# A fused attention and two-mixer kernel: the weight product on other steps with a buffer of its own, four weight pieces before the first step, VectorE's mixer work on other steps

## What is computed

```
attention: 8 heads of width 64
  scores = q k^T / 8, causal; bias = min(cum_k - cum_q, 0), cum = cumsum(max(s, 0))
  x = softmax(scores + bias) v                       -> 576 x 512 per batch
first mixer:
  gate = sigmoid(5-tap causal convolution of x over tokens)
  x = (gate * (x w_val)) w_out
second mixer:
  h = relu(x w_in); u, v = halves of h
  v_n = (v - mean v) / sqrt(var v + 1e-6)            (over the 512 features)
  out = (u * (w_spatial v_n + b_spatial)) w_out2
```

## Time and profile before

| what | value |
|---|---|
| median of the three runs | 577.82 us |
| the profiled execution | 578.55 us |
| its span, first to last instruction | 576.7 us |
| outside the span | 1.85 us |
| mean granted TensorE clock | 0.967 |
| ScalarE / VectorE / GpSimd busy | 57% / 63% / 44% of the span |
| first score matmul starts | 11.31 us |
| head 10 starts (step 50) | 155.9 us |
| the last batch is alone on the core from about | 505 us |

### The profile page before, as it was taken

The page is one execution under the profiler, slowest core; times in us unless marked ns, Lnnn a source line. Parts: engine busy times, 40 slices in busy tenths (PEclk is TensorE's granted clock), DMA queues, the critical chain, the costliest instruction groups (busy, mean ns, idle before and its releaser), DMA issues.

```text
span 576.7 us, 10409 instructions
## 1 busy us (share of the span) xinstructions
PE 519.3 (90%) x3472; PEld 453.6 (79%) x3472; DVE 365.4 (63%) x726; ACT 329.7 (57%) x844; POOL 254.8 (44%) x247
## 2 busy tenths in 40 slices
PE   1378887876999899999999999999998999999998
PEld 1256665654897699998986899988876999997997
DVE  5355766887767756676767666759576656565240
ACT  2466765675566565576665655666665645633322
POOL 2444643435457654633656635334666444003000
PEclk9998889975899999999999999999999999999999
DMA  5765454332333333344333222343333320200002
GB/s 138 215 185 142 136 135 107 83 97 70 85 84 83 84 84 78 77 114 115 96 86 84 73 72 57 93 136 95 84 91 76 84 63 13 73 20 2 1 2 82
DMA packets 46887, 50.34 MB, mean 87 GB/s; under 512 B 24881, under 2 KB 29137, under 8 KB 46834
## 3 DMA queue, kind: packets, MB, share of 16 engines
q1 hardware_dynamic: 46834, 49.68, 32.7%
HBM read 25.83 MB, written 4.95 MB: 53 GB/s over the span
## 4 chain that ended last, share of the span: by engine, by line
PE 44%; DVE 4%; ACT 2%; issue 1%; POOL 1%; DMA 0%; ACTq 0%; SPq 0%; POOLq 0%
PE mix L1039 23%; PE attn_o L1007 5%; PE attn_o L1039 4%; PE score L1039 4%; PE turned L998 3%; PE score L977 2%; PE score L978 1%; DVE u_t L895 1%; DVE neg_max L849 1%; DVE u_t L933 1%; PE score L979 1%; DVE pt_lo L867 1%; PE score L986 1%; PE score L987 1%; DVE stats L925 1%
## 5 line engine op out<-in xcount | busy, mean ns | idle before, releaser
L721 ACT ACTIVATE prob<-score,neg_max 128x128 f32<-128x128 f32 (+4 forms) x159 | 90.3, 568 | 108.7 <-DVE neg_max L849 108.2
L867 DVE TENSOR_TENSOR pt_lo<-turned,pt_hi 128x128 fp32r<-128x128 f32 (+4 forms) x160 | 77.5, 489 | 67.2 <-ACT pt_hi L730 66.5
L849 DVE TENSOR_REDUCE neg_max<-score 128x1 f32<-128x128 f32 (+4 forms) x159 | 85.1, 535 | 38.1 <-PE score L979 32.1
L730 ACT ACTIVATE pt_hi<-turned 128x128 fp32r<-128x128 f32 (+4 forms) x160 | 66.6, 435 | 42.2 <-PE turned L998 40.7
L634 POOL TENSOR_TENSOR q<-raw,raw_hi 64x576 fp32r<-64x576 f32 x32 | 46.0, 1438 | 86.3 <-issue 69.4
L977 PE MATMUL score<-k,q 68*128 68x256 f32 (+2 forms) x128 | 54.3, 424 | 29.3 <-ACT prob L721 14.4
L998 PE MATMUL turned<-ident,prob 128*128 128x128 f32 (+1 forms) x480 | 73.6, 276 | 7.1 <-DVE pt_lo L867 7.1
L1007 PE MATMUL attn_o<-pt_hi,v_hl 128*128 128x256 f32 (+2 forms) x224 | 66.7, 314 | 6.2 <-DVE pt_lo L867 6.2
L998 PEld LDWEIGHTS turned<-ident,prob 128*128 128x128 f32 (+1 forms) x480 | 50.0, 150 | 15.7 <-issue 14.5
L406 POOL TENSOR_TENSOR act_b<-u_t,act_b 128x288 fp32r<-128x288 f32 x48 | 41.1, 860 | 42.7 <-ACT act_b L795 42.1
L1039 PE MATMUL mix<-ws_hl,act_a 128*128 128x288 f32 (+1 forms) x405 | 59.2, 298 | 0.0
(11 more groups left out here) (150 smaller groups left out, 1039.0 us busy)
## 6 DMA issues: line engine op xcount, KB each, us to landing
q<-raw_hi SPq DMA_DIRECT2D x64, 144.0 KB
k<-raw_hi SPq DMA_DIRECT2D x64, 144.0 KB
raw<-in_q SPq DMA_DIRECT2D x32, 144.0 KB, 2.7
raw<-in_k SPq DMA_DIRECT2D x32, 144.0 KB, 2.8
r_bc<-r_dram SPq DMA_DIRECT2D x32, 144.0 KB, 2.9
out<-work SPq DMA_DIRECT2D x32, 144.0 KB, 1.8
v_raw<-in_v SPq DMA_DIRECT2D x32, 128.0 KB, 2.2
u_t<-in_moe_w_in SPq DMA_DIRECT2D x7, 256.0 KB, 3.5
```

The costliest lines, as they stand in the source:

```text
L721: act.activation(prob_view(i), score_view(g, i), ACT.Exp, bias=neg_max[p][0:rows[i], i:i + 1], accum_out=row_sum[p][0:rows[i], i:i + 1]).t ...
L730: act.activation(pt_view(pt_hi, i), turned_view((g + i) % 2, i), ACT.Copy).then_inc(pt_hi_done, 1)
L849: dve.tensor_reduce(neg_max[g % 2][0:rows[i], i:i + 1], score_view(g, i), AX_X, ALU.max, negate=True).then_inc(max_done, 1)
L867: dve.tensor_tensor(pt_view(pt_lo, i), turned_view((g + i) % 2, i), pt_view(pt_hi, i).bitcast(F32), ALU.subtract).then_inc(pt_lo_done, 1)
```

## The change

1. **Weight product.** w_out now goes into `ws_hl`, the buffer of w_spatial, and `act_a` is free for x_hi, whose wait for the product is gone. The 32 parts stand on a list of steps, 6, 7, 9, 11, and then every step from 12 to 47 but i = 0 and step 17.
2. **Weights.** w_spatial's five pieces go behind the product, with w_out2's four, to steps 48 to 56 (low parts one step later), in four staging tiles used in turn. The first four pieces are loaded right behind the load of head 0 (`first_weights`), and split before step 0; `more_weights` now loads seven pieces instead of four. The bias row is rounded at step 7 instead of 3.
3. **scale_q** of a head moves one step later, from i = 4 to i = 0 of the next head.
4. **Mixer tables.** Taps, tanh, x_hi, statistics, normalisation and splits of v have other steps, and the eviction of v moves from the lead to the tail of its step.

```diff
@@ -44,17 +44,16 @@
     def put(at, step, *unit):
         at.setdefault(length + step, []).append(unit)
 
-    for n, step in enumerate((-14, -12, -11, -9, -7, -7, -6, -4, -3, -2, -1, -1, 1, 2, 3) if first else
-                             (-22, -21, -19, -17, -16, -12, -11, -9, -7, -6, -2, -1, 1, 2, 3)):
-        put(tail, step, "tap", n // TAPS, n % TAPS)
-    for t, step in enumerate((7, 7, 8, 9, 9)):
-        put(tail, step, "tap", 3, t)
-    for c, step in enumerate((-4, -1, 4, 10)):
-        put(lead, step + 1, "tanh", c)
-    for c, step in enumerate((0, 2, 4, 6)):
+    for c, step in enumerate((1, 3, 4, 6)):
         put(lead, step, "x_hi", c)
         put(tail, step, "x_lo", c)
-
+    for n, step in enumerate((-17, -16, -16, -14, -12, -11, -11, -9, -7, -6, -2, -2, -1, 1, 3) if first else
+                             (-22, -21, -21, -17, -16, -12, -11, -11, -9, -7, -2, -2, -1, 1, 3)):
+        put(tail, step, "tap", n // TAPS, n % TAPS)
+    for t, step in enumerate((7, 8, 8, 9, 9)):
+        put(tail, step, "tap", 3, t)
+    for c, step in enumerate((-5, -4, 5, 10)):
+        put(lead, step, "tanh", c)
     step = 8
     for side in range(2):
         for m in range(4):
@@ -65,10 +64,10 @@
     for j in range(5):
         put(lead, step, "mm", ("v", j, 0), 0)
         put(lead, step + 1, "mm", ("v", j, 0), 1)
-        put(lead, step + 1, "evict", ("v", j, 0))
-        put(tail, (17, 19, 21, 23, 26)[j], "stats", j)
-        put(tail, (19, 21, 23, 24, 28)[j], "norm", j)
-        put(tail, (20, 22, 24, 26, 29)[j], "split", ("v", j, 0))
+        put(tail, step + 1, "evict", ("v", j, 0))
+        put(tail, (18, 21, 22, 24, 26)[j], "stats", j)
+        put(tail, (21, 23, 24, 26, 28)[j], "norm", j)
+        put(tail, (23, 24, 25, 28, 29)[j], "split", ("v", j, 0))
         step += 2
     for n, u_step in enumerate((0, 0, 1, 2, 3, 4, 5, 5)):
         side, m = divmod(n, 4)
@@ -303,25 +302,26 @@
                 PIECES.append((view[:, k, :], P, length, to, k * length))
 
         for kk in range(NC):
-            PIECES.append((wo_view[:, kk, :], P, C, act_a, kk * C))
+            PIECES.append((wo_view[:, kk, :], P, C, ws_hl, kk * C))
             PIECES.append((wi_view[:, kk, C:2 * C], P, C, act_b, kk * C))
         cut_by(wi_view[:, :, 0:C], NC, C, w2_hl)
         WV_PIECE = len(PIECES)
         cut_by(wv_view, NC, C, wv_hl)
+        LATE_PIECE = len(PIECES)
         cut_by(w_spatial[0:FULL * P, :].rearrange("(k p) t -> p k t", p=P), FULL, S, ws_hl)
         PIECES.append((w_spatial[FULL * P:S, :], LAST, S, ws_hl, FULL * S))
-        W2_PIECE = len(PIECES)
         cut_by(w2_view, NC, C, w2_hl)
         NCOMB = 2 * NC
         STAGES = SLOTS + 2
         FIRST_LOADS = 4
         WEIGHTS_FROM = 2
-        COMB_FROM = 8
-        W2_FROM = COMB_FROM + NC * NCOMB
+        COMB_STEPS = [6, 7, 9, 11] + [n for n in range(12, H * NT + 8) if n % NT != 0 and n != 17]
+        assert len(COMB_STEPS) == NC * NCOMB
+        LATE_FROM = H * NT + 8
 
         def staged(n):
             _, r, length, _, _ = PIECES[n]
-            tile = n % STAGES if n < W2_PIECE else (SLOTS, SLOTS + 1, SLOTS - 1, SLOTS - 2)[n - W2_PIECE]
+            tile = n % STAGES if n < LATE_PIECE else (SLOTS, SLOTS + 1, SLOTS - 1, SLOTS - 2)[(n - LATE_PIECE) % 4]
             return u_t[0:r, tile, 0:length] if tile < SLOTS else work[tile - SLOTS][0:r, 0:length]
 
         block = ctx.enter_context(nc.Block())
@@ -422,16 +422,16 @@
                         call(unit[0], b, b == B - 1, *unit[1:])
 
             def weights(step):
-                for n in range(len(PIECES)):
-                    at = WEIGHTS_FROM + n if n < W2_PIECE else W2_FROM + n - W2_PIECE
+                for n in range(FIRST_LOADS, len(PIECES)):
+                    at = WEIGHTS_FROM + n if n < LATE_PIECE else LATE_FROM + n - LATE_PIECE
                     if step == at:
                         call("weights_hi", n)
                     if step == at + 1:
                         call("weights_lo", n)
 
             def comb(step):
-                n, kk = divmod(step - COMB_FROM, NC)
-                if 0 <= n < NCOMB:
+                if step in COMB_STEPS:
+                    n, kk = divmod(COMB_STEPS.index(step), NC)
                     call("comb_mm", n, kk)
                     if kk == NC - 1:
                         call("comb_evict", n)
@@ -464,15 +464,13 @@
                     call("invert_sums", g - 1)
                 if i == 0 and 0 <= g - 2 < NH:
                     call("combine", g - 2)
-                if step == 0:
-                    call("scale_q", 1)
+                if i == 0 and g + 1 < NH:
+                    call("scale_q", g + 1)
                 if i == (0 if g == 0 else 1) and g + 1 < NH:
                     call("split_qk", g + 1)
                     call("place_qk", g + 1)
                 if step == 0:
                     call("more_weights")
-                if i == 4 and g + 2 < NH:
-                    call("scale_q", g + 2)
                 if i == 2 and g + 2 < NH:
                     call("load_qk", g + 2)
                 if i == 3 and 0 <= g - 1 < NH:
@@ -486,6 +484,7 @@
 
             call("setup")
             call("load_qk", 0)
+            call("first_weights")
             call("cumulate")
             call("scale_q", 0)
             call("keep_cumulated")
@@ -494,13 +493,16 @@
             call("load_qk", 1)
             call("later_setup")
             call("load_v", 0)
+            for n in range(FIRST_LOADS):
+                call("weights_hi", n)
+                call("weights_lo", n)
             for step in range((B - 1) * H * NT + H * NT + length):
                 mixer(0, step)
                 comb(step)
                 attention(step)
                 early(step + 1)
                 weights(step)
-                if step == 3:
+                if step == 7:
                     call("bias_rows")
                 mixer(1, step)
 
@@ -520,19 +522,19 @@
                     sp.wait_ge(cum_split, n + 1)
                     sp.dma_start(cum_dram[:, n, :], words(t[1][0:NH, :])).then_inc(stored, 16)
 
-            def later_setup():
+            def first_weights():
                 for n in range(FIRST_LOADS):
                     load_weights(n)
 
             def more_weights():
-                for n in range(FIRST_LOADS, STAGES):
+                for n in range(FIRST_LOADS, FIRST_LOADS - 1 + STAGES):
                     load_weights(n)
                 sp.dma_start(r_bc[0:1, :], b_spatial.rearrange("(a t) -> a t", a=1)).then_inc(b_loaded, 16)
 
             def load_weights(n):
                 view, r, length, _, _ = PIECES[n]
-                if n >= W2_PIECE:
-                    wait_pieces(sp, W2_PIECE)
+                if n >= LATE_PIECE:
+                    wait_pieces(sp, max(LATE_PIECE, n - 3))
                 elif n >= STAGES:
                     wait_pieces(sp, n - STAGES + 1)
                 sp.dma_start(staged(n), view).then_inc(w_loaded[n % STAGES], 16)
@@ -546,11 +548,13 @@
 
             def weights_lo(n):
 
-                if 0 < n <= W2_PIECE - STAGES:
+                if FIRST_LOADS <= n <= LATE_PIECE - STAGES:
                     load_weights(n - 1 + STAGES)
-                if n == W2_PIECE - 1:
-                    for late in range(W2_PIECE, len(PIECES)):
+                if n == LATE_PIECE - 1:
+                    for late in range(LATE_PIECE, LATE_PIECE + 4):
                         load_weights(late)
+                if LATE_PIECE <= n < len(PIECES) - 4:
+                    load_weights(n + 4)
 
             def load_qk(g):
                 wait(sp, lo_made, 2 * g)
...
@@ -691,7 +695,7 @@
                 act.wait_ge(w_loaded[n % STAGES], 16 * (n // STAGES + 1))
                 if n == WV_PIECE:
                     act.wait_ge(b_placed, 32)
-                if n == W2_PIECE:
+                if n == LATE_PIECE:
                     act.wait_ge(comb_done, NCOMB)
                 act.activation(to[0:r, 0, at:at + length], staged(n), ACT.Copy).then_inc(w_hi_done, 1)
 
@@ -742,8 +746,6 @@
 
             def x_hi(b, alone, n):
                 act.wait_ge(x_done, NC * b + n + 1)
-                if b == 0 and n == 0:
-                    act.wait_ge(comb_done, NCOMB)
                 if b > 0:
                     act.wait_ge(unit_done, NU * (b - 1) + LAST_SPATIAL + 1)
                 act.activation(chan(act_a, 0, n), x_t[:, n, PAD:PAD + S], ACT.Copy).then_inc(x_hi_done, 1)
@@ -885,7 +887,7 @@
                     dve.wait_ge(x_done, NC * b + n + 1)
                     dve.wait_ge(const_loaded, 16)
 
-                    wait_pieces(dve, W2_PIECE if b == 0 else len(PIECES))
+                    wait_pieces(dve, LATE_PIECE if b == 0 else len(PIECES))
                     if NC * b + n >= SLOTS:
                         before, m = divmod(NC * b + n - SLOTS, NC)
                         dve.wait_ge(lo_done, NS * before + SPLIT[("spatial", m, 1)] + 1)
@@ -954,7 +956,7 @@
```

(6 more changed lines are left out.)

4 lines of the change are left out of this document (2 added, 2 removed).

## The result

The changed kernel takes 578.88 us (median of 20 runs, 576.69 to 581.61), the kernel before, on the same chips, 575.98 (20 runs, 574.70 to 580.02). The ratio of after to before is 1.0041, interval [1.0023, 1.0059]. The forecast was 566.0 with 557 to 575: the time lies outside it. By the bound of 1% the change makes no difference; inside that bound it is slower rather than faster. The same file run again later in the study gave 1.0020 [0.9996, 1.0043].

A forecast was written before the change was run, and what follows sets the result against it. TensorE was taken as the bound from head 12 on, and the ring of scores to transposes in the first 156 us. Terms -1.5, -4.0, -5.7, +1.2 and -2.5 sum to -12.5: 578.55 to 566.0 us, range 557 to 575.

The forecast's parts named there:

- The batches from head 12 on: Three batches: TensorE's waits at the v units shrink, a new one comes; net -0.8 us each, -2.5 in all.
- The new wait on the eviction of v tile 4: Step 66 of each batch: second u product waits 1.3 us for ScalarE's eviction behind the attention, scores queued behind it.
- Heads 2 to 7: Weight pieces, waits of q's scaling and some product parts leave these heads: -4.0 us (0 to -8).
- The rival of a falling clock: Heads 4 to 7: thinned product lets TensorE's clock fall, +18 us in place of -4.0, total 588.0; chance 0.07.
- Heads 8 and 9: Both at head 5's 12.4 us plus two val products, 28.2 in place of 33.9: -5.7 us (-2 to -9).
- "more than that" rival: Clock stays at its upper level, heads 2 to 9 all run like head 5: -15.6 us there, total 560.1; chance 0.20.
- The late pieces: Heads 9 to 11: nine pieces in steps 48 to 57 make TensorE wait now and then, +1.2 us (0 to 5.5).
- the late pieces hold VectorE: Heads 9 to 11: POOL's five pieces each hold VectorE, +5.5 us in place of +1.2, total 570.3; chance 0.15.
- the ring: Loop of scores, row maximum, exponential and transposes, said to set the pace in the first 156 us.
- The start: Heads 0 and 1: bias row's wait goes, head 2's load becomes late; row maximum near 27, -1.5 us (-4 to +1).
- The sum: Whole kernel: -1.5 - 4.0 - 5.7 + 1.2 - 2.5 = -12.5 us, from 578.55 to 566.0.
- The signs: Right: head 8 under 14 us, 9 under 15.5, 12 starting near 173. Wrong: head 10 over 16.5, a batch over 122.

The follow-up runs named there:

- e6: The changed kernel with the eviction of v back in the lead of its step: 573.50 us, 0.9955 of the kernel before.
- e9: The changed kernel with three of the seven pieces and the bias row loaded at step 3, behind head 2's q and k: 577.79 us, 1.0011.
- e1: The changed kernel with the product's parts of steps 6, 7, 9 and 11 moved to steps 15, 17, 20 and 25: 573.33 us, 0.9939.
- e2: The changed kernel with seven of nine late pieces rounded and split over 16 columns only, so its result is not right: 572.59 us, 0.9929.
- e5: The changed kernel with the product at steps 8 to 39 and the late pieces at 40 to 48: 572.15 us, 0.9934.
- e7: The kernel before with tables, scale_q and start changed, but product and w_spatial's pieces where they were: 577.48 us, 1.0022.
- e12: The kernel before with the new mixer tables alone, but v evicted in the lead as before: 575.27 us, 0.9963.
- e4: The kernel before with only the scaling of q moved one step later: 579.47 us, 1.0049.
- e3: The kernel before with the new mixer tables alone, eviction of v in the tail: 584.43 us, 1.0134.
- e13: The kernel before with the new mixer tables and the scaling of q at i = 0, nothing else: 577.42 us, 1.0010.
- e8: The kernel before with only the four early pieces, seven loads at step 0 and the bias row at step 7: 578.74 us, 1.0043.
- e10: The changed kernel with product at steps 10 to 41, late pieces at 42 to 50, v evicted in the lead, q and k loaded ahead of three pieces: 566.93 us, 0.9819.

## Why the forecast was wrong

The total was forecast at -12.5 us; the medians say +2.9, the ratio +2.4 (+1.3 to +3.4). Point by point, in the forecast's own parts:

**The batches from head 12 on: right in kind.** The new wait on the eviction of v tile 4 was named and sized at 1.3 us; the first reads 1.68, the others 1.2. The net of -0.8 a batch reads -0.8 in the second and -1.1 in the third. My own terms (-1.0, half of -1.9, +1.3) give -0.65, so the close agreement is partly luck. The first came out at +1.6 against a forecast of -0.8: it starts with a stretch at the lower clock from 182 to 186 us, as the second profile of the same file, e6 and e9 do. In e1, e2, e5 and e7 the stretch of lower clock is missing, and the group takes 120.7 or 120.8. The wait of 2.2 us on an exponential ahead of it is no explanation, since e1 has it too (2.25). What sets it off I can't say from these runs. What I had not seen is how much better the same tables do without the late eviction (e6, -1.5 a batch; e12, -9.2 in all).

**Heads 2 to 7: right, and undersized.** Forecast -4.0, measured -7.6 and -6.1. The move of scale_q alone gives -3.7 there (e4), but beside the new tables it gives next to nothing (83.4 in e3, 83.2 in e13); most of the gain comes with the move of the product and the pieces (82.6 in e7, 76.7 in after). In the working, half of what stands between head 3 and head 5 is 1.6 and not 1.3; with 0.9 for head 4 the term stays where it was. The rival of a falling clock is out: heads 4 to 7 read 1.00.

**Heads 8 and 9: the step that failed most.** The forecast said "I take both at head 5's 12.4", -5.7 us. They took 34.0 (33.9 before), at 0.75 of the granted clock. The clock stayed down from 118 to 121, 128 to 138 and 141 to 145 us. Running both heads at head 5's length and running them at full clock were told as one term, as if the extra product parts would bring the clock with them; in head 8 TensorE was busy for 12.2 of 15.4 us and still read 0.75. Nor did I name what came ahead of the val products: at 137.71 ScalarE's x_hi waited 2.58 us for GpSimd's x_t, which I had listed only against the "more than that" rival. Identical code in these heads gave 34.0 and 32.9 us, and nearly identical code 31.7, 30.5, 30.3 and 33.2 (e1, e2, e6, e9). The windows of heads 8 and 9 of after and of e6:

```profile
116.80:150.80 34.00, 29.18 (x149) 24.02 (x149) 24.52 (x43) 19.44 (x48) 13.93 (x9) 0.75 0.29 75
```

```profile
119.80:150.10 30.30, 25.31 (x148) 20.47 (x149) 23.11 (x43) 19.35 (x48) 13.96 (x9) 0.89 0.33 85
```

TensorE is not busy for 4.8 us in the one and 5.0 in the other, and for 5.0 to 5.2 in the four others. What differs is the granted clock: 0.75 goes with 34.0 us, 0.79 with 32.9 and 33.2, 0.84 with 31.7, 0.89 with 30.5 and 30.3. So the clock moves this group by up to 3.7 us under the same code. The kernel before has 0.65 there and 7.9 us not busy, so both the waits and the clock did get better; after is no shorter all the same, with 149 matmuls there in place of some 130. A term of -5.7 there could not be had on the evidence; -1 to -2 is what the mean of the six, 32.1, says.

**The late pieces: mechanism right, size wrong.** Forecast +1.2 with 5.5 as the upper bound; heads 10 and 11 take 4.7 more, and e2 and e5 give back 6.5 and 6.2 us by the ratio, 4.2 and 4.1 of it in these two heads. The rival "the late pieces hold VectorE" was the truer one here. I took the low end because "this stretch had no wait at all". That was the wrong reading: a stretch with TensorE at 14.2 of 14.2 is one where each delay of the ring shows at once, and it has nothing in hand. Timeline of head 9's end in the changed kernel:

```profile
148.70 2.42 POOL L370 TENSOR_TENSOR ws_hl<-work,ws_hl 128x576 fp32r<-128x576 f32 x1
149.02 2.71 DVE L897 SCALAR_TENSOR_TENSOR u_t<-x_t,taps,u_t 128x576 f32<-128x576 f32 x2
149.13 0.74 ACT L725 ACTIVATE prob<-score,neg_max 64x576 f32<-64x576 f32 x1 [2.40 <-DVE neg_max L851]
```

GpSimd's low part takes 2.42 us (1.40 at its shortest) and the two taps beside it 2.71. The Trainium skill ("SBUF — State Buffer", "Who interferes with whom") has an exclusive lock here, in which the first to start keeps the ports and only the second waits. The trace agrees that they collide: from 148.70 to 151.73 are 3.03 us, which is what the three take one after another (1.40 and twice 0.8, the length of a tap by itself). It doesn't agree that one of them goes free: both rows are longer than by themselves, so a late piece costs on both engines.

**The start: sign wrong.** Forecast -1.5, measured +2.4 and +3.5 (head 0 begins 0.7 to 0.9 later, heads 0 and 1 take 1.7 to 2.6 more). In the first profile the row maximum came at 27.35 against "near 27", but that was luck: my own terms, 20 and 6.5 and 1, add to 27.5 for the scaling and not to 26.5, which puts the row maximum at 28. The second profile has it at 28.00, e6 at 27.73, e1 at 28.21, e5 at 28.61: nearly nothing against 28.48. Nor is the wait on the bias row gone "whole"; VectorE waits 1.93 us for the row four steps later. What failed besides is that I counted the early parts of the product only in heads 2 to 7, as work of 0.76 us each, and gave those at steps 9 and 11 no wait. Each needs the low part of a piece that VectorE's order places only one step before it, behind row maxima, behind the wait for k, and at step 9 behind the bias row as well. They wait 4.2 and 3.3 us, with scores behind them on TensorE. e1 takes them out and gains 5.9 us in all. The bounds of the term, -4 to +1, held only its DMA side; e8 shows that this side alone is at or past the upper one (heads 0 and 1 +0.5, their beginning +1.0, ratio 1.0043), and so does e7, with the scaling at its new place (+1.4 to the end of head 1). With the early parts the same stretch takes 2.4, 3.5, 4.4, 3.4 and 1.8 us more than before (after, its second profile, e2, e6, e9); with none ahead of step 8 it takes 0.5, 1.4, 1.5 and 0.9 more (e1, e7, e8, e5). So about 1 us of the loss is the start's own and some 2 are the early parts'.

**The sum.** By the first profile: start +2.4, heads 2 to 7 -7.6, heads 8 and 9 +0.1, heads 10 and 11 +4.7, batches and rest -0.3, together -0.7. The forecast's five were -1.5, -4.0, -5.7, +1.2 and -2.5. So +3.9, -3.6, +5.8, +3.5 and +2.2 are the errors, 11.8 in all. The other 3.6 between -0.7 and +2.9 is no effect of the change but the place of the two profiled executions in their kernels' runs: before's lies 2.6 above its median, after's 1.1 below. I had taken the former as 0.7 above the median of three runs, so the base of the sum stood 2.6 us too high against the median of twenty, and by itself that put the forecast nearer to the result, not further off.

**By the ratios.** Start alone +2.5 us, tables and scale_q together +0.6, all three +1.3 (1.0022). Adding the product with its pieces leaves the kernel between 1.0020 and 1.0041, so the part meant as the core of the change is worth about nothing as it stands: what it earns in heads 2 to 7 (82.6 us in e7, 76.7 in after) it pays in heads 10 and 11 and in waits at steps 9 and 11. e5 shows that the same move earns with other steps: product from 8 to 39, pieces from 40, and 0.9934 where e7 has 1.0022, 5.1 us. e10, with product from 10 to 41 and pieces from 42, and two more edits, bears it out.

**The signs.** ScalarE's wait on r_bc is gone, and the waits of a batch are near the 2 us named (2.4 in the second). Against it: head 8 took 15.4 and not under 14, head 9 18.6 and not under 15.5, head 12 began at 182.8 and not near 173, head 10 stood at 16.5 with the limit at 16.5, and the first batch took 122.6, past the 122 that was to mean a wrong forecast.

**What stays open:** why heads 8 and 9 and the first batch are shorter in e1, where they have the same code; what sets the clock's low stretches in heads 8 and 9 and at head 12; and which of e10's three edits carries how much, since it was run only as a whole. Against the changed kernel's 1.0041 the gains of e6 (0.0086), e5 (0.0107) and e9 (0.0030) add up to 0.0223, e10's is 0.0222. Against its second measurement, 1.0020, they add up to 0.0160 and e10's is 0.0201, so the close agreement is no proof that the parts simply add.

## What to carry to other kernels

When work is moved into a queue that executes in order, price it by its latest input and by what stands behind it, not by its duration: TensorE waited 4.2 us for a product part of 0.76, with scores behind it. A stretch in which the bounding engine never waits has nothing in hand to absorb a delay: side work cost 4 to 5 us there, and two heads earlier, where TensorE waited anyway, at most some 2. When the clock of a stretch is not steady, give its term a range as wide as the clock makes it: here 3.7 us of 34. And when a table of positions is changed together with another edit, run each alone and both together: here two losses of 1.3% and 0.5% made zero, and one line of the table held the whole loss.

## What the runs showed of the hardware

An instruction of VectorE that reads two tiles can lose to several of GpSimd's in a row, not to one only. Timeline of e10:

```profile
143.74 3.77 DVE L370 TENSOR_TENSOR w_hl<-work,w_hl 128x512 fp32r<-128x512 f32 x1
```

```profile
142.58 1.53 POOL L370 TENSOR_TENSOR ws_hl<-work,ws_hl 64x576 fp32r<-64x576 f32 x1
144.08 0.87 POOL L657 TENSOR_TENSOR v_hl<-v_raw,v_hl 128x320 fp32r<-128x320 f32 x1
144.92 0.79 POOL L406 TENSOR_TENSOR act_b<-u_t,act_b 128x288 fp32r<-128x288 f32 x1
145.67 1.28 POOL L370 TENSOR_TENSOR w_hl<-u_t,w_hl 128x512 fp32r<-128x512 f32 x1
```

A subtraction that takes 0.67 us by itself took 3.77: it began while the first of four GpSimd instructions ran, and ended 0.56 us after the fourth, which ended at 146.95. GpSimd's four stand back to back, and the last takes 1.28, as low parts of that size do elsewhere (1.27 at 32.02 in the changed kernel). So in this place the price of side work on GpSimd was the length of its whole chain, with VectorE's ring behind it. The row maximum behind that subtraction came at 149.37, and ScalarE waited 5.64 us for it: e10 has time left there.

The scaling of q, with one input tile, was lengthened too, from 0.45 to 1.50 us beside GpSimd (e4).

The same code at another granted clock is another time: six profiles of heads 8 and 9 with nearly the same work took 30.3 to 34.0 us at 0.89 to 0.75, with TensorE not busy for 4.8 to 5.2 us in all of them.
